# Reordering the first batch of an attention and feed-forward kernel: weight splits and loads tied to slots

## The chip, the cores and the metric

One core of a Trainium2 chip runs the program. The metric is the device time of that core in microseconds (us). Below, PE is TensorE, DVE is VectorE, ACT is ScalarE, POOL is GpSimd, and SP is the SyncE queue that issues every DMA of this kernel.

## The reference

All data are float32. Attention works on q, k, v of shape (4, 8, 576, 64) at two scales and adds the results; two feed-forward layers follow on x of shape (2304, 512).

```python
# coarse: mean over 4 neighbours of q, k and v, full softmax attention on 144 tokens, each row repeated 4 times
out_up = repeat(softmax(scale * q_d @ k_d.T) @ v_d, 4)
# local: softmax over the keys with |i - j| < 4
out_local = softmax(where(mask, scale * q @ k.T, -1e9)) @ v
x = (out_up + out_local)                 # to (2304, 512)
h = x @ w_in1;  y = maximum(0.01 * h, h) @ w_out1
h = y @ w_in2;  out = (h - tanh(h)) @ w_out2      # w_in 512 x 2048, w_out 2048 x 512
```

## The kernel before

**Pairs of heads.** The 32 heads form 16 pairs. One pair's attention is cut into 17 steps, 0 to 16, each a few instructions on each engine (the functions `attention` of the five blocks). Steps 0 to 3 transpose q and k on PE and copy them to SBUF on ACT; step 4 puts the mask and the local scores into two PSUM banks (PE), and DVE takes the maximum of the first; step 5 subtracts the maxima (DVE), and its first subtraction frees bank 0; step 6 is the coarse scores (PE) and the sum of v over 4 neighbours (POOL, three additions, `vd`); step 7 is the maximum of the coarse scores (DVE) and the exponential of the local ones (ACT, L679); step 8 the coarse exponential (ACT, L683) and the local row sums (DVE, L944 to L948); steps 9 and 10 the multiplications by 1/sum (POOL, L1112 and L1117); steps 11 to 14 transpose the probabilities (PE, L451, L456) and copy them (ACT, for some DVE); steps 15 and 16 are the products with v (PE), and DVE adds the two scales into xT.

**The first batch.** Before any feed-forward work can start, the four pairs A, B, C and D4 (written D in the text) of batch 0 run together. Each has a place for its tiles and two PSUM banks. The generator `batch0` (L260) writes out their order on every engine: in slot t pair A is at step t, B at step t-4, C at t-8, D at t-12; within a slot the steps below 6 come first, then falling step numbers. A dictionary, another one for each engine, moves single steps: `(A, 6): (B, 3)` puts A's step 6 behind B's step 3. A name such as C4 below is step 4 of pair C. Every engine works in order, so this order is what an instruction can be stuck behind; semaphores guard the tiles and banks.

**Feed-forward layer 1.** It runs over 8 tiles of 288 tokens. In each tile f runs over 16 slices of 128 hidden units: `hidden1` is w_in times x, `down1` is w_out times the activation, two slices behind. Each product is three float32r products of high and low parts (hi*hi, hi*lo, lo*hi). The high part of a weight is a copy by ACT (`split_kept`, L708), the low part a subtraction by POOL (L1121). Slices 0 to 7 (`KEPT`) are split once and kept, written K0 to K7 for ACT and k0 to k7 for POOL below; 8 to 15 are split again in each tile. K0 and K1 are split within the first batch (`EARLY = 2`), K2 right behind it, K3 to K7 in tile 0. The first tile's x is split too (`split_first_x` on ACT, L733, `lo_of_first_x` on DVE, L976), one part for each pair A to D. During tiles 0 to 5 the attention of two further pairs is threaded between the slices (`later`, L275), all in place A; the first of them is "pair 1" of A.

**Loads.** SP issues all loads in a fixed order (L360 to L387): q and k, v in two layouts (`v4n` for the coarse scale, `vw` for the local one), and the weight slices (`load_kept`, two DMAs of 256 KB each). `load_kept(f)` waits until POOL is done with slice f-4, and `load_whole(0)` until DVE is done with pairs C and D.

**Fillers.** PE begins with 8 throw-away matmuls (`fill`, L630), and five further places of the batch have one or two.

Of the kernel before, what the change touches and what calls it, by code (L numbers as in the profile page):

```python
# [59 lines left out]
def two_scale_attention_and_feed_forward(nc, q, k, v, w_in1, w_out1, w_in2, w_out2, out):  # L60
# [36 lines left out]
    with ExitStack() as ctx:  # L97
# [161 lines left out]

        def batch0(behind):  # L260

            def placed(at, s):
                yield at, s
                for (moved, step), place in behind.items():
                    if place == (s, at):
                        yield from placed(step, moved)

            for slot in range(STEPS + 3 * BEHIND):
                places = [(slot - BEHIND * c, s) for c, s in enumerate(FIRST)
                          if 0 <= slot - BEHIND * c < STEPS]  # L270
                for at, s in sorted(places, key=lambda place: (place[0] % STEPS >= 6, -(place[0] % STEPS))):
                    if (s, at) not in behind:
                        yield from placed(at, s)

        def later(f, tile, last):  # L275

# [34 lines left out]
        def _(sp):  # L311
# [62 lines left out]
            load_qk(A, 1, 8)  # L374
            load_kept(2)
# [40 lines left out]
        def _(pe):  # L416
# [246 lines left out]
        def _(act):  # L663
# [185 lines left out]
            act.wait_ge(band_copied, 1)  # L849
            copy_band(top, 2, NB - 1, 1).then_inc(band_copied, 1)  # L850
            act.wait_ge(zeros_set, 1)
            for step, s in batch0({(A, 8): (C, 1), (A, 11): (B, 7), (A, 12): (B, 8), (A, 15): (C, 8), (B, 11): (C, 7), (B, 12): (C, 8),
                                   (D4, 7): (B, 14), (C, 15): (D4, 11)}):
                attention(step, s, 0)
                if (s, step) == (B, 7):
                    split_kept(0)
                elif (s, step) == (D4, 8):
                    split_kept(1)
                elif (s, step) == (D4, 11):
                    split_first_x(0)  # L860
                elif (s, step) == (D4, 13):
                    split_first_x(1)
                elif (s, step) == (D4, 15):
                    split_first_x(2)
# [26 lines left out]
        def _(dve):  # L891
# [171 lines left out]
            last.then_inc(zeros_set, 1)  # L1063
            dve.wait_ge(zeros_set, 1)
            dve.wait_ge(band_copied, 2)
            for step, s in batch0({(A, 8): (B, 5), (B, 8): (C, 5), (C, 12): (D4, 8), (D4, 9): (C, 12),
                                   (A, 15): (C, 14), (A, 16): (A, 15), (B, 15): (D4, 12), (B, 16): (B, 15),
                                   (C, 15): (B, 16), (C, 16): (D4, 14)}):
                attention(step, s, 0, 0, FIRST.index(s))
                if (s, step) == (D4, 15):  # L1070
                    lo_of_first_x(0)
                    lo_of_first_x(1)
            lo_of_first_x(2)
# [22 lines left out]
        def _(pool):  # L1096
# [129 lines left out]
```

## Time and profile before

| What | Value |
| --- | --- |
| time, median of 3 runs | 953.15 us (952.77 to 954.95) |
| the profiled execution | 954.95 us, its span 953.2 us |
| PE busy | 940.0 us (99% of the span) |
| DVE, ACT, POOL busy | 538.8, 558.4, 403.3 us |
| DMA over the span | 41.48 MB, mean 44 GB/s |
| DMA over the first 60 us | 11.25 MB, mean 188 GB/s |

The span begins with the first recorded instruction. A busy engine is not an engine at its peak, and a share over the whole span says little on the first 70 us, where the change is; the rows are therefore taken from there.

### The profile page before, as it was taken

How to read it: one execution, taken by the hardware profiler on the slowest of the kernel's cores; microseconds unless marked ns; L12 is line 12 of the kernel's file. 1: busy time of each engine (PE TensorE's matmuls, PEld its weight loads, DVE VectorE, ACT ScalarE, POOL GpSimd, SP SyncE). 2: the span in 40 equal slices, each digit the busy share in tenths (PEclk: the TensorE clock that was granted, in tenths of full speed). 3: DMA queues.
4: the chain of work that ended last, by engine and by line, in shares of the span. 5: the costliest groups of instructions: out<-in, count | busy, mean ns of one | idle time of the engine just before them, and what ended most of it. 6: DMA issues, size and time to landing. Idle time of an engine off the chain costs nothing.

```text
span 953.2 us, 19930 instructions
## 1 busy us (share of the span) xinstructions
PE 940.0 (99%) x7026; PEld 883.5 (93%) x7026; DVE 538.8 (57%) x1078; ACT 558.4 (59%) x1351; POOL 403.3 (42%) x343
## 2 busy tenths in 40 slices
PE   8989999999999999999999999999999999999998
PEld 8789999999999999999999989899899898898997
DVE  6745445534544554453236576776666766766764
ACT  5655546445445455464446687666666756756754
POOL 4675517227245155171433667332233233233232
PEclk9999999999999999999999999999999999999999
DMA  7785111210221121102004012000000000000000
GB/s 160 178 209 140 39 39 28 51 32 20 49 51 26 25 51 36 41 3 67 1 2 128 17 57 88 21 14 1 34 0 0 33 0 0 33 0 0 34 1 33
DMA packets 87797, 41.48 MB, mean 44 GB/s; under 512 B 60352, under 2 KB 81344, under 8 KB 87744
## 3 DMA queue, kind: packets, MB, share of 16 engines
q1 hardware_dynamic: 87744, 40.78, 16.4%
q8 instruction: 33, 0.54, 0.2%
q14 instruction: 20, 0.16, 0.1%
HBM read 36.04 MB, written 4.72 MB: 43 GB/s over the span
## 4 chain that ended last, share of the span: by engine, by line
PE 88%; POOL 3%; ACT 3%; DMA 2%; issue 1%; SPq 1%; DVE 1%; ACTq 0%; POOLq 0%; DVEq 0%
PE ph L538 13%; PE ph L539 13%; PE ph L540 13%; PE acc L567 7%; PE acc L568 7%; PE acc L569 7%; PE acc L614 6%; PE acc L615 6%; PE acc L616 6%; PE banks L427 2%; PE banks L464 2%; PE banks L420 1%; POOL g_lo L1149 1%; PE banks L451 1%; POOL w_lo_b L1156 1%
## 5 line engine op out<-in xcount | busy, mean ns | idle before, releaser
L1149 POOL TENSOR_TENSOR g_lo<-scratch,g_hi 128x384 fp32r<-128x384 f32 x96 | 125.6, 1308 | 258.1 <-ACT g_hi L741 258.1
L996 DVE TENSOR_TENSOR ph<-g,ph 128x288 f32<-128x288 f32 x128 | 59.1, 462 | 169.2 <-ACT g L755 168.6
L538 PE MATMUL ph<-x_hi,w_hi_a 128*128 128x288 f32 (+1 forms) x448 | 143.7, 321 | 0.2
L540 PE MATMUL ph<-x_hi,w_lo_a 128*128 128x288 f32 (+1 forms) x448 | 140.0, 312 | 0.0
L539 PE MATMUL ph<-x_lo,w_hi_a 128*128 128x288 f32 (+1 forms) x448 | 139.9, 312 | 0.0
L1128 POOL TENSOR_TENSOR in_lo<-w_whole,in_hi 128x512 fp32r<-128x512 f32 x64 | 82.5, 1289 | 132.3 <-ACT in_hi L721 131.5
L755 ACT ACTIVATE g<-ph 128x288 f32<-128x288 f32 x128 | 52.6, 411 | 134.5 <-PE ph L540 134.5
L1133 POOL TENSOR_TENSOR out_lo<-w_whole,out_hi 128x512 fp32r<-128x512 f32 x64 | 86.2, 1347 | 71.8 <-ACT out_hi L725 71.7
L1030 DVE SCALAR_TENSOR_TENSOR scratch<-scratch,ph 128x384 f32<-128x384 f32 x96 | 53.2, 554 | 108.9 <-ACT scratch L804 104.3
L803 ACT ACTIVATE scratch<-ph 128x384 f32<-128x384 f32 x96 | 46.8, 488 | 108.2 <-PE ph L540 106.7
L983 DVE TENSOR_TENSOR g_lo<-ph,g_hi 128x288 fp32r<-128x288 f32 x128 | 58.6, 458 | 59.3 <-ACT g_hi L741 59.3
L538 PEld LDWEIGHTS ph<-x_hi,w_hi_a 128*128 128x128 f32 x448 | 84.3, 188 | 3.3 <-issue 0.6
L539 PEld LDWEIGHTS ph<-x_lo,w_hi_a 128*128 128x128 f32 x448 | 84.2, 188 | 1.4
L540 PEld LDWEIGHTS ph<-x_hi,w_lo_a 128*128 128x128 f32 x448 | 84.2, 188 | 0.0
L538 PE MATMUL ph<-x_hi,in_hi 128*128 128x288 f32 x256 | 79.1, 309 | 0.0
L567 PE MATMUL acc<-g_hi,out_hi 128*128 128x288 f32 x256 | 76.9, 300 | 0.5 <-POOL out_lo L1133 0.5
L568 PE MATMUL acc<-g_lo,w_hi_a 128*128 128x288 f32 x256 | 75.7, 296 | 0.0
L568 PE MATMUL acc<-g_lo,out_hi 128*128 128x288 f32 x256 | 75.7, 296 | 0.0
L569 PE MATMUL acc<-g_hi,out_lo 128*128 128x288 f32 x256 | 75.7, 296 | 0.0
L567 PE MATMUL acc<-g_hi,w_hi_a 128*128 128x288 f32 x256 | 75.6, 295 | 0.0
L539 PE MATMUL ph<-x_lo,in_hi 128*128 128x288 f32 x256 | 75.5, 295 | 0.0
L569 PE MATMUL acc<-g_hi,w_lo_a 128*128 128x288 f32 x256 | 75.5, 295 | 0.0
(273 smaller groups left out, 2638.1 us busy)
## 6 DMA issues: line engine op xcount, KB each, us to landing
out_dram<-o_stage SPq DMA_DIRECT2D x18, 256.0 KB, 2.0
w_whole<-in_moe_w_in_dram SPq DMA_DIRECT2D x16, 256.0 KB, 4.2
w_whole<-in_moe_w_out_dram SPq DMA_DIRECT2D x16, 256.0 KB, 5.1
qn<-in_q_dram SPq DMA_DIRECT2D x26, 144.0 KB
kn<-in_k_dram SPq DMA_DIRECT2D x26, 144.0 KB
v4n<-in_v_dram SPq DMA_DIRECT2D x26, 144.0 KB
vw<-in_v_dram SPq DMA_DIRECT2D x26, 122.5 KB
scratch<-in_moe_w_in_dram SPq DMA_DIRECT2D x8, 256.0 KB, 2.8
```

Source lines behind the costliest of these rows:

```text
L538: pe.matmul(bank, whi, x_hi[:, c, 0:width], start=(c == 0), stop=False)
L539: pe.matmul(bank, whi, x_lo[:, c, 0:width], start=False, stop=False)
L540: last = pe.matmul(bank, wlo, x_hi[:, c, 0:width], start=False, stop=(c == CD - 1))
L567: pe.matmul(acc[:, c, 0:T1], whi, g1_hi[:, f % 3, :], start=(f == 0), stop=False)
L568: pe.matmul(acc[:, c, 0:T1], whi, g1_lo[:, f % 3, :], start=False, stop=False)
L569: last = pe.matmul(acc[:, c, 0:T1], wlo, g1_hi[:, f % 3, :], start=False, stop=(f == CF - 1))
L614: pe.matmul(acc[:, j, 0:DM], hi, whi, start=(f == 0), stop=False)
L983: dve.tensor_tensor(g1_lo[:, f % 3, :], ph1[:, 1 - f % 2, 0:T1], g1_hi[:, f % 3, :].bitcast(F32), ALU.subtract).then_inc(g_lo_done, 1)
L996: dve.tensor_tensor(ph1[:, 1 - f % 2, 0:T1], g1[:, f % 2, :], ph1[:, 1 - f % 2, 0:T1], ALU.max)\
L1128: pool.tensor_tensor(in_lo[:, f % 2, :], w_whole[:, f - KEPT, 0:DM], in_hi[:, f % 2, :].bitcast(F32), ALU.subtract).then_inc(in_lo_done, 1)
L1133: pool.tensor_tensor(out_lo[:, f % 2, :], w_whole[:, f - KEPT, DM:CW], out_hi[:, f % 2, :].bitcast(F32), ALU.subtract).then_inc(out_lo_don ...
L1149: pool.tensor_tensor(g2_lo[:, f % 3, :], g2[:, f % 2, :], g2_hi[:, f % 3, :].bitcast(F32), ALU.subtract).then_inc(g_lo_done, 1)
```

## The change

The dictionaries of PE, ACT, DVE and POOL lose most of their entries, `batch0` yields the slot number as well, and the splits of K0 and K1, k0 and k1, and of the first x are tied to the beginning of slots. SP issues the first two weight slices later. The fillers are the same, at the same steps.

```diff
+KEPT_HI_SLOTS = (22, 26)
+KEPT_LO_SLOTS = (24, 27)
+FILL = {("a", 1): 2, ("a", 3): 2, ("b", 1): 1, ("b", 3): 2, ("c", 3): 2}
+X_HI_SLOTS = {27: (0, 1), 28: (2,)}
+X_LO_SLOTS = {27: (0, 1), 28: (2,)}
@@ SP
             load_v4(B, 0, 2)
-            load_kept(0)
             load_qk(D4, 0, 6)
-            load_vw(A, 0, 0)
             load_v4(C, 0, 4)
             load_v4(D4, 0, 6)
+            load_vw(A, 0, 0)
             load_vw(B, 0, 2)
+            load_kept(0)
+            load_vw(C, 0, 4)
             load_kept(1)
-            load_vw(C, 0, 4)
             load_vw(D4, 0, 6)
@@ PE
-            for step, s in batch0({(A, 6): (B, 3), (B, 6): (C, 3), (C, 6): (D4, 3), (A, 11): (C, 4), (A, 15): (D4, 4),
-                                   (B, 11): (D4, 4), (C, 15): (D4, 12), (C, 16): (D4, 14)}):
+            for _, step, s, i in batch0({(A, 11): (C, 4), (B, 11): (D4, 4), (C, 15): (D4, 12), (C, 16): (D4, 14)}):
@@ ACT
-            for step, s in batch0({(A, 8): (C, 1), (A, 11): (B, 7), (A, 12): (B, 8), (A, 15): (C, 8), (B, 11): (C, 7), (B, 12): (C, 8),
-                                   (D4, 7): (B, 14), (C, 15): (D4, 11)}):
-                attention(step, s, 0)
-                if (s, step) == (B, 7):
-                    split_kept(0)
-                elif (s, step) == (D4, 8):
-                    split_kept(1)
-                elif (s, step) == (D4, 11):
-                    split_first_x(0)
...
+            for slot, step, s, i in batch0({(D4, 7): (B, 15), (C, 15): (D4, 11)}):
+                if slot != done:
+                    for c in X_HI_SLOTS.get(slot, ()):
+                        split_first_x(c)
+                if slot != done and kept_at(KEPT_HI_SLOTS, slot) is not None:
+                    split_kept(kept_at(KEPT_HI_SLOTS, slot))
+                done = slot
+                attention(step, s, i)
@@ DVE
-            for step, s in batch0({(A, 8): (B, 5), (B, 8): (C, 5), (C, 12): (D4, 8), (D4, 9): (C, 12),
-                                   (A, 15): (C, 14), (A, 16): (A, 15), (B, 15): (D4, 12), (B, 16): (B, 15),
-                                   (C, 15): (B, 16), (C, 16): (D4, 14)}):
...
+            for slot, step, s, i in batch0({(C, 12): (D4, 9), (A, 15): (C, 14), (A, 16): (A, 15),
+                                            (B, 15): (D4, 12), (B, 16): (B, 15), (C, 15): (B, 16),
+                                            (C, 16): (D4, 14)}):
@@ POOL
-            for step, s in batch0({(B, 6): (A, 6), (D4, 6): (C, 9)}):
-                attention(step, s, 0)
-                if (s, step) == (A, 10):
-                    split_kept(0)
-            for f in range(1, EARLY + 1):
-                split_kept(f)
+            for slot, step, s, i in batch0({(D4, 6): (D4, 10)}):
+                if slot != done and kept_at(KEPT_LO_SLOTS, slot) is not None:
+                    split_kept(kept_at(KEPT_LO_SLOTS, slot))
...
+            split_kept(EARLY)
```

Written out from slot 6 on, the orders are these (f: fillers; x0 to x3, l0 to l3: high and low parts of the first x):

```
PE   before: B2 B3 f A6 B4 C0 C1 C2 C3 f B6 C4 A11 D0 A12 D1 A13 D2 A14 D3 C6 D4 A15 B11 A16 B12 B13 B14 D6 B15 C11 B16 ...
PE   after:  B2 A6 B3 f B4 C0 C1 C2 B6 C3 f C4 A11 D0 A12 D1 A13 D2 A14 C6 D3 A15 D4 B11 A16 B12 B13 B14 D6 B15 C11 B16 ...
ACT  before: B3 A7 C0 C1 A8 C2 C3 B7 K0 A11 D0 B8 A12 D1 A13 D2 A14 D3 C7 B11 C8 A15 B12 B13 B14 D7 B15 C11 D8 K1 C13 D11 x0 C15 D13 x1 D15 x2 x3
ACT  after:  B3 A7 C0 A8 C1 C2 C3 A11 B7 D0 A12 B8 D1 A13 D2 A14 D3 A15 B11 C7 B12 C8 B13 B14 B15 D7 C11 D8 C13 K0 D11 C15 D13 K1 x0 x1 D15 x2 x3
DVE  before: A5 B3 A7 B4 B5 A8 A9 C3 B7 C4 C5 B8 B9 D3 C7 D4 C8 D5 C9 D7 D8 C12 D9 C14 A15 A16 D12 B15 B16 C15 D14 C16 D15 l0 l1 D16 l2 l3
DVE  after:  A5 B3 A7 B4 A8 B5 A9 C3 B7 C4 B8 C5 B9 D3 C7 D4 C8 D5 C9 D7 D8 D9 C12 C14 A15 A16 D12 B15 B16 C15 D14 C16 l0 l1 D15 l2 D16 l3
POOL before: A6 B6 A9 A10 k0 B9 B10 C6 C9 D6 C10 D9 D10 k1 k2
POOL after:  A6 A9 A10 B6 B9 B10 C6 C9 C10 D9 D10 D6 k0 k1 k2
```

## Rows read from the trace of the kernel before

**Rows 1.** Windows: us, then busy us (instructions), PE clock, DMA share, GB/s.
```profile
43.00:60.00 17.00, 16.32 (x149) 15.37 (x148) 9.94 (x21) 10.52 (x24) 10.47 (x7) 1.00 1.01 247
60.00:72.00 12.00, 9.77 (x83) 8.97 (x83) 3.95 (x9) 6.37 (x14) 8.69 (x6) 1.00 0.61 148
72.00:90.00 18.00, 18.00 (x195) 17.67 (x192) 8.85 (x19) 8.81 (x20) 10.50 (x10) 1.00 0.70 185
```
**Rows 2.** Waits of PE in 0 to 150 us: total, times, longest.
```profile
PE banks L451 <- POOL pl L1112: 2.4, 2, 1.8
...
PE banks L446 <- ACT kT L673: 0.7, 1, 0.7
...
PE banks L451 <- ACT pT L688: 0.4, 1, 0.4
```
**Rows 3.** Timeline of PE: start, length, line, operation [idle before].
```profile
5.12 1.21 PE L420 MATMUL banks<-ident,qn 72*128 72x72 f32 x8
...
13.86 0.90 PE L503 MATMUL banks<-kdT,qd_diag 128*96 128x144 f32 x6
...
16.27 0.72 PE L420 MATMUL acc<-ident,turned_c 72*128 72x72 f32 x8
...
19.66 1.38 PE L427 MATMUL acc<-kT_c,qT_c 64*64 64x70 f32 x36
21.55 0.63 PE L451 MATMUL banks<-ident,pl 128*70 128x128 f32 x4 [0.52 <-POOL pl L1112]
...
26.82 1.38 PE L427 MATMUL ph<-kT_d,qT_d 64*64 64x70 f32 x36
...
37.00 0.44 PE L456 MATMUL acc<-ident,pd_c 96*72 96x96 f32 x3 [0.42 <-DVE turned_c L957]
...
42.49 0.72 PE L420 MATMUL banks<-ident,qn 72*128 72x72 f32 x8
```
**Rows 4.** Timeline of DVE, columns as in Rows 3.
```profile
13.11 0.51 DVE L929 TENSOR_TENSOR pl<-banks,mxl 128x350 f32<-128x350 f32 x1
...
17.64 0.51 DVE L929 TENSOR_TENSOR xT<-acc,xT 128x350 f32<-128x350 f32 x1
...
18.92 0.80 DVE L944 TENSOR_REDUCE rs<-pl 128x9 f32<-128x630 f32 x1
...
29.53 0.80 DVE L944 TENSOR_REDUCE rs_c<-pl_c 128x9 f32<-128x630 f32 x1
```
**Rows 5.** Timeline of ACT.
```profile
19.10 0.73 ACT L679 ACTIVATE xT<-xT 128x630 f32<-128x630 f32 x1
...
26.23 0.76 ACT L679 ACTIVATE pl_c<-pl_c 128x630 f32<-128x630 f32 x1
...
45.34 1.06 ACT L710 ACTIVATE w_hi_a<-w_whole 128x1024 fp32r<-128x1024 f32 x1 [0.71 <-DMA w_whole<-in_moe_w_out_dram]
...
53.27 1.06 ACT L710 ACTIVATE w_hi_a<-w_whole 128x1024 fp32r<-128x1024 f32 x1 [2.31 <-DMA w_whole<-in_moe_w_out_dram]
...
64.27 1.06 ACT L710 ACTIVATE w_hi_a<-w_whole 128x1024 fp32r<-128x1024 f32 x1 [4.29 <-DMA w_whole<-in_moe_w_out_dram]
```
**Rows 6.** Timeline of POOL.
```profile
22.32 2.36 POOL L1123 TENSOR_TENSOR w_lo_a<-w_whole,w_hi_a 128x1024 fp32r<-128x1024 f32 x1
...
32.97 1.53 POOL L1105 TENSOR_TENSOR vd_d<-vd_d,v4n_d 72x256 f32<-72x256 f32 x2
...
61.16 1.24 POOL L1112 TENSOR_TENSOR pl<-pl,rs 128x630 f32<-128x630 f32 x1
```
**Rows 7.** Timeline of the SP queue: issue start, length.
```profile
13.48 0.41 SPq L344 DMA_DIRECT2D w_whole<-in_moe_w_in_dram  x1
...
16.18 2.63 SPq L317 DMA_DIRECT2D turned_d<-in_k_dram  x2
...
36.00 1.72 SPq L315 DMA_DIRECT2D qn<-in_q_dram  x2
...
56.66 0.87 SPq L346 DMA_DIRECT2D w_whole<-in_moe_w_out_dram  x1
```

More of the change, by code:

```diff
@@ L85, in two_scale_attention_and_feed_forward @@
     WHOLE = CF - KEPT
+    EARLY = len(KEPT_HI_SLOTS)
     assert D == QB and DM == CD * P and LP * RUN == S and NB * QB == S and PAIRS == 4 + 2 * MIXED
@@ L260, in batch0, with placed @@
         def batch0(behind):
-            def placed(at, s):
-                yield at, s
+            def placed(slot, at, s):
+                yield slot, at, s, 0
                 for (moved, step), place in behind.items():
                     if place == (s, at):
-                        yield from placed(step, moved)
+                        yield from placed(slot, step, moved)
             for slot in range(STEPS + 3 * BEHIND):
@@ L272, in batch0, with kept_at @@
                     if (s, at) not in behind:
-                        yield from placed(at, s)
+                        yield from placed(slot, at, s)
+        def kept_at(slots, slot):
+            return slots.index(slot) if slot in slots else None
         def later(f, tile, last):
@@ L636, in _ @@
             fill(8, ph1[:, 1, :])
-            fills = {(A, 1): 2, (A, 3): 2, (B, 1): 1, (B, 3): 2, (C, 3): 2}
-            for step, s in batch0({(A, 6): (B, 3), (B, 6): (C, 3), (C, 6): (D4, 3), (A, 11): (C, 4), (A, 15): (D4, 4),
-                                   (B, 11): (D4, 4), (C, 15): (D4, 12), (C, 16): (D4, 14)}):
-                attention(step, s, 0)
-                fill(fills.get((s, step), 0), ph1[:, 1, :])
+            for _, step, s, i in batch0({(A, 11): (C, 4), (B, 11): (D4, 4), (C, 15): (D4, 12), (C, 16): (D4, 14)}):
+                attention(step, s, i)
+                fill(FILL.get(("abcd"[FIRST.index(s)], step), 0), ph1[:, 1, :])
             for step in range(HEAD):
@@ L851, in _ @@
             act.wait_ge(zeros_set, 1)
-            for step, s in batch0({(A, 8): (C, 1), (A, 11): (B, 7), (A, 12): (B, 8), (A, 15): (C, 8), (B, 11): (C, 7), (B, 12): (C, 8),
-                                   (D4, 7): (B, 14), (C, 15): (D4, 11)}):
-                attention(step, s, 0)
-                if (s, step) == (B, 7):
-                    split_kept(0)
-                elif (s, step) == (D4, 8):
-                    split_kept(1)
-                elif (s, step) == (D4, 11):
-                    split_first_x(0)
[L861 to L864, printed above, removed]
+            done = -1
+            for slot, step, s, i in batch0({(D4, 7): (B, 15), (C, 15): (D4, 11)}):
[5 more added lines that the diff above has]
+                done = slot
+                attention(step, s, i)
             split_first_x(CD - 1)
@@ L1065, in _ @@
             dve.wait_ge(band_copied, 2)
-            for step, s in batch0({(A, 8): (B, 5), (B, 8): (C, 5), (C, 12): (D4, 8), (D4, 9): (C, 12),
-                                   (A, 15): (C, 14), (A, 16): (A, 15), (B, 15): (D4, 12), (B, 16): (B, 15),
-                                   (C, 15): (B, 16), (C, 16): (D4, 14)}):
[L1069 to L1073, printed above, removed]
+            done = -1
+            for slot, step, s, i in batch0({(C, 12): (D4, 9), (A, 15): (C, 14), (A, 16): (A, 15),
+                                            (B, 15): (D4, 12), (B, 16): (B, 15), (C, 15): (B, 16),
+                                            (C, 16): (D4, 14)}):
+                if slot != done:
+                    for c in X_LO_SLOTS.get(slot, ()):
+                        lo_of_first_x(c)
+                done = slot
+                attention(step, s, i, i, FIRST.index(s))
             lo_of_first_x(CD - 1)
@@ L1183, in _ @@
                 pool.memset(s.vw[:, 0:NB:NB - 1, :, :], 0.0).then_inc(vw_zeroed, 1)
-            for step, s in batch0({(B, 6): (A, 6), (D4, 6): (C, 9)}):
-                attention(step, s, 0)
-                if (s, step) == (A, 10):
-                    split_kept(0)
-            for f in range(1, EARLY + 1):
-                split_kept(f)
+            done = -1
+            for slot, step, s, i in batch0({(D4, 6): (D4, 10)}):
+                if slot != done and kept_at(KEPT_LO_SLOTS, slot) is not None:
+                    split_kept(kept_at(KEPT_LO_SLOTS, slot))
+                done = slot
+                attention(step, s, i)
+            split_kept(EARLY)
             layer1(0, CF)
```

1 line of the change is left out of this document (removed).

## The prediction

> **What bounds the kernel now.** I began with the table by windows, since a share over 953 us can't speak for an edit to the first 43. From 72 us on PE is busy without a hole (18.00 of 18.00), at a granted clock of 1.00, the 2.4 GHz level [rows 1]. Whatever comes out of the change must therefore move the moment at which PE enters this dense run. Then the waits of PE, to see what stands before it. Behind the first batch there are three: 0.7 for a copy of k, 1.8 for a multiplication by POOL, 0.4 for a copy of the probabilities, 2.9 us together [rows 2]; the windows agree (0.7 idle in 43 to 60, 2.2 in 60 to 72). Last the timelines, for what these waits hang on: ACT is in order, and its splits K2, K4 and K6 start when their DMA has landed, at 45.34, 53.27 and 64.27, after 0.71, 2.31 and 4.29 us of idleness [rows 5]. The DMA engines are full from 43 to 60 (share 1.01, 247 GB/s) [rows 1]. So the kernel has two racing paths to about 67 us: the first batch on the engines, and the weights through SP and DMA. The second one ends last; the first has some slack. That is the hinge of this prediction.
>
> **The change in the first batch.** I follow the new order with the lengths of the rows; ends and starts are some 0.05 to 0.15 us apart, as between 13.11 + 0.51 = 13.62 [rows 4] and the start at 13.86 behind the fillers.
>
> Step 1, A6 ahead of B3 on PE. A6 waits for the first subtraction of A5, which ends at 13.62 [rows 4]; it used to wait behind B3 and two fillers instead. It starts near 13.7, takes 0.65, then come B3 (0.25) and the fillers (0.5), so B4 starts at 15.1, and C0, which stood at 16.27 [rows 3], at 16.9: 0.6 late. DVE's B4 is late by 0.5 with it.
>
> Step 2, A8 ahead of B5 on DVE, and B6 ahead of C3 on PE. A8 (sum, epsilon, reciprocal, 1.26 us) runs from 18.1 instead of 18.92 [rows 4], so POOL can multiply 0.8 earlier. But B5's first subtraction goes from 17.64 [rows 4] to 19.3, it ends at 19.8, and it frees the bank that B6 waits for. PE has done C2 at 18.0 and stands at B6 until 19.9, with C3, the fillers and C4 queued behind. C3 ends at 20.8, the fillers at 21.3, and C4's masks and scores (1.8) at 23.1, against 19.66 + 1.31 = 20.97 before [rows 3]: 2.1 late. A11 follows at 23.1 instead of 21.55 [rows 3].
>
> Step 3, ACT. The exponential B7, at 19.10 before [rows 5], now stands behind A11 and runs from 24.1 to 24.8. DVE's B8 waits for it until 24.9 and C5, now behind B8, runs from 26.1; C6 on PE then from 26.7. ACT's D3 comes at 28.0, D4's scores on PE from 29.3 to 30.6, against 26.82 to 28.12 [rows 3]. The exponential C7, 26.23 before [rows 5], now stands behind B11, which needs PE after D4: it ends at 32.4, and DVE's C8 starts at 32.5 against 29.53 [rows 4], 2.9 late. D5, D7, D8 follow; DVE's copy C12, now behind D9, starts at 38.8, and PE's C14, which waits for it, at 39.5 against 37.00 [rows 3]. From there the order on PE is the old one, so that pair 1's A0, 42.49 before [rows 3], comes at about 45.0. The delay at the end of the batch is 2.5 us.
>
> Bounds of this step: the order removes nothing from any engine. PE's waits inside the batch are the ceiling of a gain: 0.52 and 0.42 in the rows and some 2.7 in all by its timeline, so -2.7. Above, the stalls of steps 1 to 3 with no overlap add up to 0.6 + 1.9 + 0.6 + 0.7 + 1.1 = 4.9. I take 2.5, the walk.
>
> Step 4, the tail. POOL's D6 (0.7 + 1.53 [rows 6]) moves behind D10; PE's D15 waits for it. D10 ends at 40.4 in the walk, D6 at 42.7, and D15 is due at 43.3: hidden by 0.6. k0 (2.36 [rows 6]) then ends at 45.1 and k1 at 47.5; the first slice on PE is due at 45.5 and ends when the last low part of x is ready, near 47.1, the second is due at 48.1: hidden by 0.4 and 0.6. K0, K1 and the x parts fill holes of ACT, except K1 ahead of x0, which is hidden because x3 waits for D16 anyway.
>
> Step 5, the loads. SP issues without a pause, so the same issues in another order reach A's next q at 36.00 [rows 7] again. K0, issued at 13.48 [rows 7], goes to about 27.5 and K1 to 31.8; ACT needs them at 39 and 42.6 now. D's q and k land earlier, but PE's D0 stands behind A11 and gains nothing. Vw of A is issued some 0.7 later and needed at 28, by A15. Cost zero; bounds -1 to +1, since a pair of like issues took 2.63 us at 16.18 and 1.72 at 36.00 [rows 7]: the queue can back up by 0.9 in one place, and the order decides where. The waits of later loads hold too: the fifth kept slice needs k0 by 47, which is done at 45.1.
>
> **What the DMA path absorbs.** ACT's K2 waits 0.71 for its DMA [rows 5], so a delay of 2.5 is 1.8 to 1.9 from there on, and PE's wait of 0.7 [rows 2] is its mirror. At K4 ACT has 2.31 of idleness [rows 5]: all 1.9 is swallowed on ACT. On DVE it is not: pair 1's A4 and A5 end 1.9 later, at 55.7, and the activation maximum that stood at 54.66 now waits for them, 1.0 late. That runs on through the coarse maximum, ACT, k5 and POOL's multiplication at 61.16 [rows 6], so that PE's A11 starts 1.0 after its old 62.5. PE itself arrives there at 62.4, so it waits 1.1 instead of 1.8. Then A13: before, it waited 0.4 for a copy that stood behind K6 on ACT, itself held by the landing at 64.25 of the DMA issued at 56.66 [rows 2, 5, 7]. This landing doesn't move. PE comes 1.0 late and 0.4 is absorbed: 0.6 us enters the dense run, and there is no slack in it to take it away or add to it.
>
> The sum: 2.5 - 0.7 - 0.8 - 0.4 = +0.6 us. On the profiled execution's own 954.95 (span 953.2 and 1.75 around it) that is 955.55; that execution was 1.8 above the median of the runs, so I set it on the median, 953.15 + 0.6 = 953.8. More generally the result is the delay of the batch less about 2, and never below zero unless the DMA comes earlier.
>
> **A rule of the skill.** Across the wait of 1.8 at 60.6 [rows 2] the granted clock stays 1.00 [rows 1], though the eight transposes at 5.12 took 1.21 us and the like ones at 16.27 took 0.72 [rows 3], so PE did begin slower than it goes on. The Trainium skill, "TensorE: Matmul & The Clock Gate", Part 1 (The HAM clock gate), says that activity releases the throttle and that idleness brings it back, half the pace. By that rule the new stall in front of B6 could do harm well beyond its length; by the row of the wait at 60.6, of the same length, it does none. The sum goes by the row.
>
> **The rivals.**
> (a) PE falls back to the slow pace behind the new stalls (18.0 to 19.9, and again near 26 and 38). For: the slow first transposes; the new stalls stand closer together than any before. Against: the wait of 1.8 did no harm. Place: C3 to B11, some 10 us of PE; at 1.21 against 0.72 [rows 3] the work of about 6 us grows by 4, the batch is 6.5 late, and the total +4.5: 957.6. It decides from a batch delay of 4 on, below that the waits for DMA take it up.
> (b) The reorder pays: POOL, DVE and the earlier loads of v and D overlap better than I see, and the batch is not late. For: A8 is 0.8 earlier. Against: B6's bank. Time: nothing is gained, since A13 still waits for K6: 953.15, within 0.2%.
> (c) DMA comes earlier: the kept slices out of the congested early queue make SP quicker, K4 and K6 land up to 2 us earlier, and the batch isn't late. The most that can go are the 2.9 us of waits [rows 2]: 950.3. Against: the engines are full from 43 to 60, and SP's issues are the same.
> (d) The queue backs up more, or the new tail on POOL (D6, k0, k1 in a row) shows: each further microsecond there goes straight to the first slices. With 2 more the batch is 4.5 late: +2.6, 955.7.
>
> **How the numbers follow.** A difference of 0.2%, 1.9 us, is about what a measurement of this kernel tells from none. The forecast (a delay of 1.5 to 3.8 at the batch's end, 0 to +1.8 in total) gets 0.53, (b) 0.15, (a) 0.07, (d) 0.14, (c) 0.11. (d) and (a) are slower by over 0.2% but for 0.02 of (d): 0.19. (c) is faster by over 0.2%: 0.11, less 0.01 of it that falls short: 0.10. Same: 0.71. The range reaches from 951.3, within (c), to 956.8, past (d); the likeliest case alone is 953.15 to 955.0.
>
> **What would show it.** In the changed kernel's timeline PE waits some 1.9 us before B6 near 18 to 20; DVE's B8 and C8 wait for ACT's exponential; A0 of pair 1 starts near 45. K4 and K6 still start at 53.3 and 64.3 after DMA; PE's wait for POOL's multiplication shrinks from 1.8 to about 1.1, the two others to nothing, and from 72 us on PE is dense. The prediction is wrong if K6 starts more than 1 us off 64.3, if A0 comes before 43 or after 46.5, or if a wait of PE appears behind 72 us.

## The result and the profile after

The changed kernel takes 959.66 us (median, 958.63 to 960.50), the kernel before beside it on the same chips 953.55 (952.77 to 954.95): a ratio of 1.0062 with a 95% interval of [1.0044, 1.0080]. The prediction said 953.8 with a range up to 956.8. The profiled execution took 958.32, its span is 956.5.

The windows (length, then busy us (instructions) of PE, PEld, DVE, ACT and POOL, PE clock, DMA share, GB/s), two of the first batch and the three of [rows 1]:

```profile
12.00:20.00 8.00, 6.04 (x74) 5.40 (x75) 6.96 (x16) 3.35 (x12) 3.84 (x5) 0.93 0.93 171
20.00:28.00 8.00, 7.06 (x82) 6.21 (x80) 5.45 (x14) 4.52 (x16) 3.87 (x5) 0.85 0.89 153
...
43.00:60.00 17.00, 15.07 (x190) 14.21 (x190) 12.83 (x25) 9.92 (x23) 12.26 (x9) 0.90 1.00 284
60.00:72.00 12.00, 11.81 (x93) 11.56 (x92) 5.97 (x13) 8.28 (x20) 10.84 (x6) 1.00 0.47 117
72.00:90.00 18.00, 18.00 (x199) 17.50 (x198) 6.66 (x14) 8.73 (x21) 8.37 (x8) 1.00 0.56 160
```

From 72 us on nothing has changed in kind: 18.00 of 18.00 busy, clock 1.00. What changed lies before. In 12 to 28 and in 43 to 60 the mean granted clock is below 1, so a part of each stretch was spent at 1.2 GHz.

The waits of PE (total, times, longest), against [rows 2]:

```profile
PE ph L546 <- DVE xT L897: 1.9, 1, 1.9
PE acc L464 <- DVE turned_c L959: 1.9, 1, 1.9
PE acc L511 <- DVE xT L931: 1.6, 1, 1.6
```

The three long waits of before, for kT, pl and pT, are gone or are 0.2 us. In their place stand B6 (L511), C14 (L464) and the first slice of layer 1 (L546). They are in the timeline of PE, which answers to [rows 3]:

```profile
5.12 0.75 PE L428 MATMUL banks<-ident,qn 72*128 72x72 f32 x8
...
15.37 0.72 PE L428 MATMUL acc<-ident,turned_c 72*128 72x72 f32 x8
...
18.49 1.32 PE L511 MATMUL acc<-xT 128*96 128x144 f32 x6 [1.62 <-DVE xT L931]
...
21.69 1.66 PE L435 MATMUL acc<-kT_c,qT_c 64*64 64x70 f32 x36
23.29 0.63 PE L459 MATMUL banks<-ident,pl 128*70 128x128 f32 x4
...
29.61 1.38 PE L435 MATMUL ph<-kT_d,qT_d 64*64 64x70 f32 x36
...
40.89 0.44 PE L464 MATMUL acc<-ident,pd_c 96*72 96x96 f32 x3 [1.88 <-DVE turned_c L959]
...
46.39 0.72 PE L428 MATMUL banks<-ident,qn 72*128 72x72 f32 x8
49.04 0.40 PE L546 MATMUL ph<-x_hi,w_hi_a 128*128 128x288 f32 x1 [1.93 <-DVE xT L897]
...
67.01 1.07 PE L459 MATMUL banks<-ident,pl 128*70 128x128 f32 x8 [0.19 <-POOL pl L1115]
71.10 0.27 PE L459 MATMUL banks<-ident,pl 128*70 128x128 f32 x1
```

C0 starts at 15.37, 0.9 earlier than in the trace of before. That is not the order's doing: kernels that are the same up to there have it at 15.37 (the change) and 17.31 (fill_three below), since PE's first transposes and fillers ran slowly for a shorter or a longer time (0.75 for the first transposes in the change, 1.21 or 1.22 in before and fill_three). Stretches are therefore counted from C0. From there to pair 1's A0, at 46.39, PE needs 31.02 us instead of 26.22. The last row, step A13 at 71.10, opens the dense run: in this and every other trace of the study the span ends 885.2 to 886.7 us behind A13. So one moment carries the whole result, and the experiments are read by it.

DVE and ACT show what the waits hang on:

```profile
39.00 1.05 DVE L954 TENSOR_SCALAR rs_d<-rs_d 96x3 f32<-96x3 f32 x1 [0.29 <-ACT pd_d L689]
...
40.18 0.66 DVE L959 COPY turned_c<-acc 70x512 f32<-70x512 f32 x1
...
45.50 3.35 DVE L980 TENSOR_TENSOR x_lo<-xT,x_hi 128x288 fp32r<-128x288 f32 x2
```
```profile
24.45 0.72 ACT L685 ACTIVATE xT<-xT 128x630 f32<-128x630 f32 x1
...
32.08 0.72 ACT L685 ACTIVATE pl_c<-pl_c 128x630 f32<-128x630 f32 x1
...
56.20 1.05 ACT L716 ACTIVATE w_hi_a<-w_whole 128x1024 fp32r<-128x1024 f32 x1
...
64.40 1.05 ACT L716 ACTIVATE w_hi_a<-w_whole 128x1024 fp32r<-128x1024 f32 x1
```
```profile
38.79 1.24 POOL L1115 TENSOR_TENSOR pl_d<-pl_d,rs_d 128x630 f32<-128x630 f32 x1 [2.16 <-DVE rs_d L950]
...
43.49 4.67 POOL L1126 TENSOR_TENSOR w_lo_a<-w_whole,w_hi_a 128x1024 fp32r<-128x1024 f32 x2
```

On DVE a tiny operation on 96 x 3 takes 1.05 us and ends with POOL's multiplication (40.05 and 40.03); its like in other places takes 0.20. The first two low parts of x take 3.35 while POOL computes k0 and k1, and the second of them ends at 48.85, 0.69 behind POOL's k1 (43.49 + 4.67 = 48.16). On ACT the exponentials B7 and C7 are 5.4 and 5.9 later than in [rows 5], and K4 and K6 (56.20, 64.40) no longer wait for their DMA.

### The profile page after: what moved, and what is told of

Read it like the earlier page. It is cut to its first block, busy times and chain, and to the rows that moved or that the text cites. A ratio compares the mean times of both kernels' runs of the same rounds, so it can differ in the third digit from the quotient of the medians.

```text
span 956.5 us, 19930 instructions
## 1 busy us (share of the span) xinstructions
PE 940.8 (98%) x7026; PEld 884.6 (92%) x7026; DVE 541.5 (57%) x1078; ACT 558.0 (58%) x1351; POOL 403.2 (42%) x343
## 4 chain that ended last, share of the span: by engine, by line
PE 89%; POOL 3%; ACT 3%; DMA 2%; issue 1%; DVE 1%; SPq 0%; ACTq 0%; DVEq 0%; POOLq 0%
PE ph L546 14%; PE ph L547 13%; PE ph L548 13%; PE acc L575 7%; PE acc L576 7%; PE acc L577 7%; PE acc L622 6%; PE acc L623 6%; PE acc L624 6%; PE banks L435 2%; PE banks L472 2%; PE banks L459 1%; PE banks L428 1%; POOL g_lo L1152 1%; POOL w_lo_b L1159 1%
## 5 line engine op out<-in xcount | busy, mean ns | idle before, releaser
L546 PE MATMUL ph<-x_hi,w_hi_a 128*128 128x288 f32 (+1 forms) x448 | 144.1, 322 | 2.1 <-DVE xT L897 1.9
L546 PEld LDWEIGHTS ph<-x_hi,w_hi_a 128*128 128x128 f32 x448 | 84.7, 189 | 5.2 <-DVE xT L897 2.1
L546 PE MATMUL ph<-x_hi,in_hi 128*128 128x288 f32 x256 | 79.1, 309 | 0.0
L747 ACT ACTIVATE g_hi<-ph 128x288 fp32r<-128x288 f32 x128 | 52.8, 412 | 39.2 <-DVE ph L998 36.6
```

What stands on the lines that cost most here:

```text
L546: pe.matmul(bank, whi, x_hi[:, c, 0:width], start=(c == 0), stop=False)
```

## The experiments

Executions of one kernel differ in their mean granted clock, and an execution at 0.996 or less is as a rule longer than one at 0.998 or more; between 0.998 and 1.0 the clock doesn't order the times. Where this matters the clock is given. "Orders" are the written orders of PE, ACT and DVE; "tail" is the rest: D6, k0, k1 behind D10 on POOL, the places of K0, K1 and of x, and the loads. Each ratio is against the kernel before on the same chip. The median of before differs from chip to chip (952.50 to 953.85), so times of different rows are compared by their ratios.

| run | what it is | median us (n) | ratio [95%] |
|---|---|---|---|
| core_only | before, new orders | 963.11 (6) | 1.0096 [1.0073, 1.0120] |
| tail_only | after, old orders | 954.56 (11) | 1.0013 [1.0004, 1.0021] |
| short_lo | after, k0 and k1 cut | 960.87 (6) | 1.0074 [1.0053, 1.0096] |
| fill_c2 | after, 6 fillers behind C2 | 959.85 (6) | 1.0065 [1.0050, 1.0081] |
| pe_only | before, PE's new order | 954.66 (12) | 0.9993 [0.9974, 1.0013] |
| dve_only | before, DVE's new order | 953.52 (12) | 1.0003 [0.9995, 1.0012] |
| pe_dve | before, both | 955.19 (11) | 1.0017 [1.0008, 1.0025] |
| fill_three | after, 21 fillers in three places | 957.63 (5) | 1.0040 [1.0027, 1.0053] |
| act_only | before, ACT's new order | 954.56 (11) | 1.0020 [1.0012, 1.0029] |
| act_old | after, ACT's old order | 956.28 (5) | 1.0039 [1.0026, 1.0052] |
| fill_short | fill_three, k0 and k1 cut | 956.68 (6) | 1.0044 [1.0029, 1.0060] |
| loads_early | before, other order of later loads | 952.52 (12) | 1.0006 [0.9986, 1.0026] |
| core_fill | core_only, 13 fillers in two places | 957.03 (5) | 1.0042 [1.0029, 1.0055] |
| fix_b6 | after, B6 and A8 back | 959.90 (6) | 1.0069 [1.0049, 1.0088] |
| fix_c12 | after, C12 ahead of D9 | 959.72 (6) | 1.0071 [1.0057, 1.0085] |
| tail_short | tail_only, k0 and k1 cut | 953.43 (11) | 1.0001 [0.9992, 1.0011] |
| loads_fill | loads_early, 3 fillers behind C4 | 952.34 (12) | 0.9981 [0.9962, 1.0000] |

### Orders or tail

My theory behind the result was: the orders stall PE, the stalls cost clock, and k0 and k1 hold up DVE. Rivals were the tail on POOL and the loads.

**core_only**: before.py with the three new tables of places.

```
-  ACT: batch0({(A, 8): (C, 1), (A, 11): (B, 7), ... (D4, 7): (B, 14), (C, 15): (D4, 11)})
+  ACT: batch0({(D4, 7): (B, 15), (C, 15): (D4, 11)})      and PE's and DVE's as in the change
```

> The kernel before with only the new dictionaries of PE, ACT and DVE; POOL's order, SP's loads and the places of K0, K1, the x parts stay as before. Theory 'orders' (the stalls in the batch, B6 above all, with the slow pace of PE behind them, are the loss): most of the 6.1 us, 957 to 960. Theory 'tail' (k0 and k1 late on POOL hold the low parts of x on DVE): the delay of the batch is taken up by the waits for DMA, 953 to 954.5.

**tail_only**: the change with the three old tables.

```
+  PE, ACT, DVE: the tables of before; all else as changed
```

> The changed kernel with the old dictionaries of PE, ACT and DVE: left of the change are POOL's order (D6, k0, k1 late), the slots of K0, K1, x0 to x3, l0 to l3, and SP's loads. Theory 'tail': 3 us or more slower than before, 956.5 to 959, and the two low parts of x on DVE take 3 us or more instead of 0.8. Theory 'orders': within 1 us of before, 952.5 to 954.5.

Core_only loses more than the whole change by the medians (963.11), though the two intervals overlap; tail_only loses 1.3 us, a little more than its theory 'orders' allowed. The orders are the main cause. What no expectation had is the spread of core_only: its six executions took 957.43, 958.27, 963.07, 963.16, 965.22 and 965.92 at mean clocks of 0.998, 0.996, 0.989, 0.989, 0.986 and 0.986. The only window up to 72 us in which the clock goes, in the fastest of them:

```profile
20.00:28.00 8.00, 6.67 (x75) 5.82 (x74) 5.85 (x13) 3.85 (x9) 2.39 (x3) 0.79 0.89 174
```

**short_lo**: POOL computes 64 of the 1024 columns of k0 and k1 (the other columns of these low parts are left out and are zero, which takes one memset more on POOL at the start).

```
+                cut = slice(0, 64 if f < EARLY else CW)
+                pool.tensor_tensor(w_lo_a(f, cut), w_whole[:, WHOLE - 4 + f % 4, cut], ...
```

> The changed kernel with k0 and k1 cut to 64 of 1024 columns on POOL (the rest of the two low parts is left at zero, so that part of the computation is left out). Theory 'tail': the two low parts of x take 0.8 us again instead of 3.35, the first slice of layer 1 starts 2.5 to 3 us earlier and the time is 2 to 3 us under that of the changed kernel, about 957. Theory 'orders': DVE's x parts as before, but the time moves by less than 1 us, 958.7 to 960.5.

**fill_c2**: six fillers behind C2, where PE stands before B6.

```
-FILL = {("a", 1): 2, ("a", 3): 2, ("b", 1): 1, ("b", 3): 2, ("c", 3): 2}
+FILL = {("a", 1): 2, ("a", 3): 2, ("b", 1): 1, ("b", 3): 2, ("c", 2): 6, ("c", 3): 2}
```

> The changed kernel with 6 fillers on PE behind C2, where PE otherwise waits 1.6 us for B6. Theory 'clock' (the stall there lets the clock fall, granted 0.93 and 0.85 in 12 to 28 us): the clock is 1.00 in 12 to 28 us, the batch ends 1.5 to 2.5 us earlier, and since the dense run of PE starts with it, 957.5 to 958.5. If the stalls alone cost, nothing or up to +0.3 us on 959.7.

Neither helps: short_lo lies above both branches of its expectation, fill_c2 where the stalls alone would have it. In short_lo the time again follows the clock (956.78 and 957.84 at 0.998, 960.84 and 960.90 at 0.991, 962.34 at 0.989, 964.30 at 0.986), so its median says nothing of k0 and k1. Its trace does: the low parts take 0.82, the wait before the first slice is gone, the clock is 1.00 from 43 us on, and A13 comes 21.82 behind A0 instead of 24.71. In fill_c2 the clock is 1.00 where the fillers are, and falls later:

```profile
12.00:20.00 8.00, 7.11 (x90) 6.16 (x87) 6.99 (x14) 4.39 (x14) 2.36 (x4) 1.00 0.90 184
20.00:28.00 8.00, 6.83 (x85) 5.97 (x85) 6.78 (x16) 4.11 (x14) 5.13 (x6) 1.00 0.85 143
...
36.00:43.00 7.00, 5.12 (x66) 4.25 (x67) 4.71 (x11) 4.27 (x14) 4.31 (x5) 0.89 0.76 202
43.00:52.00 9.00, 7.55 (x115) 6.20 (x113) 6.82 (x13) 4.04 (x12) 5.54 (x4) 0.90 0.77 200
```

### Which engine's order

**pe_only**, **dve_only** and **pe_dve** put one or two of the tables into the kernel before.

```
-  PE:  batch0({(A, 6): (B, 3), (B, 6): (C, 3), (C, 6): (D4, 3), (A, 11): (C, 4), (A, 15): (D4, 4), ...})
+  PE:  batch0({(A, 11): (C, 4), (B, 11): (D4, 4), (C, 15): (D4, 12), (C, 16): (D4, 14)})
```

> The kernel before with PE's new dictionary alone. DVE still does B5 ahead of A8, so B6 waits little behind C2. Theory 'order and clock' (a long stall of PE needs both orders, and the clock falls only behind a long stall): C0 and all behind it 0.6 us late, clock at least 0.998, 953 to 954.5. Theory 'PE's order alone': over 956.

```
-  DVE: batch0({(A, 8): (B, 5), (B, 8): (C, 5), (C, 12): (D4, 8), (D4, 9): (C, 12), (A, 15): (C, 14), ...})
+  DVE: batch0({(C, 12): (D4, 9), (A, 15): (C, 14), ...})
```

> The kernel before with DVE's new dictionary alone: B5 stands behind A8, and PE does C3 and the fillers before it waits for B6, so that stall is about 0.9 us. Theory 'order and clock': 953 to 955, clock at least 0.996. Theory 'DVE's order alone': over 956.

```
+  both
```

> The kernel before with the new dictionaries of PE and DVE; ACT as before, so the exponentials B7 and C7 come early. If the stall before B6 and the clock behind it are the loss: 956 to 960 with a mean clock under 0.996. If ACT's order is needed as well: 953.5 to 955.5.

**act_only** is the kernel before with ACT's new table alone, **act_old** the change with ACT's old one.

```
-  ACT: batch0({(A, 8): (C, 1), (A, 11): (B, 7), (A, 12): (B, 8), (A, 15): (C, 8), (B, 11): (C, 7), ...})
+  ACT: batch0({(D4, 7): (B, 15), (C, 15): (D4, 11)})
```

> The kernel before with ACT's new dictionary alone, so that A11's copy stands ahead of the exponential B7 and B11's ahead of C7. Theory 'ACT' (the in-order coupling of the exponentials to PE's transposes is what turns the batch late): 956 us or more and a mean clock of 0.996 or less. Theory 'coupling' (ACT's order costs only where PE's and DVE's orders have already made C4 late): 953 to 955.

```
+  the reverse, in the changed kernel
```

> The changed kernel with ACT's old dictionary. Both theories: faster than the changed kernel. By the sum of what was measured (1.7 for PE's and DVE's orders, 1.3 for the tail) 956.0 to 957.0; if ACT's order has no part, 959.7.

DVE's order alone costs nothing, PE's alone next to nothing (its interval is wide because one execution of before took 964.18, at a clock of 0.984; the medians are 1.2 apart), ACT's alone +2.1, PE's and DVE's +1.7; all three cost 9.9. They don't add up: by the medians the parts alone come to 3.3. Act_old agrees with ACT's share: at 1.0039 it is 2.3 us better than the change, give or take 1.4. (Its 956.28 lies in the expected range, but on a chip where before takes 952.50; by the ratio it is just above it.) The exponentials B7 and C7 show how the delays hang together, in pe_dve:

```profile
20.58 0.71 ACT L678 ACTIVATE xT<-xT 128x630 f32<-128x630 f32 x1
27.41 0.70 ACT L678 ACTIVATE pl_c<-pl_c 128x630 f32<-128x630 f32 x1
```

and in the changed kernel at 24.45 and 32.08. With PE's and DVE's orders, in which A8 goes ahead of B5, B7 is 1.5 later than in [rows 5]. With ACT's order too, B7 is queued behind A11, which needs PE after C4: another 3.9. In act_only, ACT's order alone puts B7 at 22.88, 3.8 later than in [rows 5]. So the delays of B7 add up (1.5 and 3.8 against 5.4), and the step from 3.3 to 9.9 us must come from elsewhere; "The clock, taken out" below finds it.

In dve_only A0 comes at 43.67 and A13 at 65.65:

```profile
43.67 0.72 PE L420 MATMUL banks<-ident,qn 72*128 72x72 f32 x8
...
65.65 0.27 PE L451 MATMUL banks<-ident,pl 128*70 128x128 f32 x1
```
```profile
62.07 1.06 ACT L710 ACTIVATE w_hi_a<-w_whole 128x1024 fp32r<-128x1024 f32 x1 [3.01 <-DMA w_whole<-in_moe_w_out_dram]
```

A0 is 1.2 later than in [rows 3] and A13 1.4 earlier, since K6, which starts when its DMA has landed, does so at 62.07 and not at 64.27. Seven traces have K6 waiting for this landing: pe_only and act_only at 62.45, tail_only 62.66 and tail_short 62.84 stand with dve_only's, pe_dve at 64.57 with that of before, although SP's order is the same in before, dve_only, pe_only, act_only and pe_dve. So the row of before that I used is one of the two late ones. Part of the lateness is there when SP issues the load: at 56.66 in before and 58.55 in pe_dve, against 55.70, 56.79 and 55.44 in dve_only, pe_only and act_only; from the issue to K6's start it is 7.6 and 6.0 against 6.4, 5.7 and 7.0. What holds the queue back, and how much of it is chance, one trace of each kernel can't tell.

### The clock, taken out

**fill_three**: fillers in all three places in which PE waits.

```
+FILL: ("c", 2): 6
+                if (s, step) == (C, 13):
+                    pe.wait_ge(D4.bank_free[1], uses1(0, 3))
+                    fill(7, ph1[:, 1, :])
+            pe.wait_ge(B.bank_free[0], uses0(1, 0))      # ahead of the first slice
+            fill(8, acc[:, 0, :])
```

> The changed kernel with fillers in all three of its long stalls of PE: 6 behind C2, 7 behind C13, 8 ahead of the first slice of layer 1. Theory 'clock': the granted clock is 1.00 in every window up to 72 us, the mean 0.998 or more in every execution, and the time falls to 954.5 to 957, what is left being the stalls themselves. Theory 'stalls': 959 to 960.5 as in the changed kernel.

**fill_short**: the same with k0 and k1 cut as in short_lo.

```
+                cut = slice(0, 64 if f < EARLY else CW)      # in fill_three
```

> The changed kernel with fillers in its three long stalls and with k0 and k1 cut to 64 of 1024 columns (the rest of these low parts is left at zero). With the clock held at its full level the effect of POOL's splits on DVE's x parts can be read: theory 'tail' says the two parts take 0.8 us instead of 3.4 and the time falls from 957.6 by 1 to 2 us, to 955.6 to 956.6. If POOL's splits don't hold DVE: 957.6.

**core_fill**: core_only with the fillers behind C2 and C13.

```
+ fills[(C, 2)] = 6, and behind C13: pe.wait_ge(D4.bank_free[1], uses1(0, 3)); fill(7, ph1[:, 1, :])
```

> The three new dictionaries alone (as core_only, 963.1) with 6 fillers behind C2 and 7 behind C13. Theory 'clock': mean clock 0.998 or more in nearly every execution and 955.5 to 957.5, so that 5 us or more of that kernel's loss is the pace. If the orders themselves cost it: 960 or more.

With fillers core_only goes from 963.11 to 957.03, its clock is 1.0 in four executions of five, and 13 useless matmuls have made the kernel 6 us faster by the medians (5 us by the ratios, give or take 3, since core_only spreads so widely). The window and A0 and A13:

```profile
20.00:28.00 8.00, 6.39 (x83) 5.37 (x82) 7.49 (x16) 5.59 (x17) 4.56 (x4) 1.00 0.90 167
```
```profile
46.41 0.72 PE L420 MATMUL banks<-ident,qn 72*128 72x72 f32 x8
...
68.24 0.27 PE L451 MATMUL banks<-ident,pl 128*70 128x128 f32 x1
```

The change itself goes from 1.0062 to 1.0040 in fill_three, 2.1 us; the difference has an uncertainty of 1.8 us, so in the change the clock's price is likely and its size open. The medians leave fill_three 0.6 above what was expected. What is left at full clock, +3.6 in core_fill and +3.8 to +4.1 in fill_three (by medians 957.63 to 953.50), is the delay proper. The 3.6 is near the 3.3 of the three tables alone: what did not add up there was the clock.

Fill_short has 1.0044, on another chip: cutting k0 and k1 shows nothing in the time there, and its expectation missed. Its trace says why it could hardly show more. The low parts are ready at 46.82, but the eight fillers now hold PE until 49.20:

```profile
47.45 2.00 PE L641 MATMUL acc<-ident 128*128 128x128 f32 x16
49.20 0.38 PE L546 MATMUL ph<-x_hi,w_hi_a 128*128 128x288 f32 x1
```

### One stall at a time

**fix_b6** puts B6 back behind C3 and A8 behind B5; **fix_c12** puts C12 back ahead of D9.

```
-  PE:  batch0({(A, 11): (C, 4), ...            DVE: batch0({(C, 12): (D4, 9), ...
+  PE:  batch0({(B, 6): (C, 3), (A, 11): (C, 4), ...    DVE: batch0({(A, 8): (B, 5), (C, 12): (D4, 9), ...
```

> The changed kernel with B6 behind C3 on PE and A8 behind B5 on DVE, as before the change, everything else changed. The stall of 1.6 us before B6 goes. Theory 'B6' (that stall and the slow pace behind it are the largest part): 956 to 957.5. Theory 'ACT chain' (the exponentials behind A11 and B11 set the pace whatever B6 does): 958.5 or more.

```
-  DVE: batch0({(C, 12): (D4, 9), ...
+  DVE: batch0({(C, 12): (D4, 8), (D4, 9): (C, 12), ...
```

> The changed kernel with DVE's copy C12 ahead of D9, as before the change. The stall of 1.9 us before C14 goes. Theory 'each stall counts' 957.5 to 958.7; if the path through the exponential D8 sets the end anyway, 959.3 to 960.

Neither is better than the change, at 1.0069 and 1.0071: the theories 'B6' and 'each stall counts' are out, and the times fall where the other branch of each expectation had them. In fix_b6 the stall before B6 is gone from the trace, and the clock is worse than ever in it:

```profile
28.00:36.00 8.00, 8.00 (x85) 6.50 (x86) 3.67 (x8) 2.42 (x7) 2.11 (x3) 0.50 0.76 199
...
43.00:52.00 9.00, 9.00 (x108) 7.88 (x106) 6.28 (x14) 3.69 (x9) 6.73 (x5) 0.54 0.76 186
52.00:60.00 8.00, 8.00 (x76) 7.79 (x75) 3.57 (x7) 5.17 (x12) 3.55 (x2) 0.67 0.93 292
```

PE is busy for all 8.00 us of 28 to 36, at half the speed (this execution took 962.42, the second longest of its six). In fix_c12 the wait before C14 falls from 1.88 to 0.42 and that before the first slice grows from 1.93 to 2.96: the stall moved.

```profile
39.35 0.44 PE L464 MATMUL acc<-ident,pd_c 96*72 96x96 f32 x3 [0.42 <-DVE turned_c L959]
...
48.97 0.41 PE L546 MATMUL ph<-x_hi,w_hi_a 128*128 128x288 f32 x1 [2.96 <-DVE xT L897]
```

DVE's low parts and POOL's k0 and k1 in the same trace:

```profile
44.36 4.42 DVE L980 TENSOR_TENSOR x_lo<-xT,x_hi 128x288 fp32r<-128x288 f32 x2
```
```profile
43.42 4.67 POOL L1126 TENSOR_TENSOR w_lo_a<-w_whole,w_hi_a 128x1024 fp32r<-128x1024 f32 x2
```

DVE began its low parts 1.1 earlier than in the change and ended them at the same moment, 48.78 against 48.85, and A13 stayed (71.04 against 71.10). The end hangs on POOL: in all seven traces with whole k0 and k1 at their new place (after, tail_only, act_old, fill_c2, fill_three, fix_b6, fix_c12) the second low part ends 0.68 or 0.69 behind k1, although A0 stands anywhere from 40.93 to 51.53. So in the change's trace the path that ends last goes through POOL: D10, D6, k0, k1, then the low parts, the first slice, A13. The end of the batch, A0, stands beside it.

### k0, k1 and DVE

**tail_short**: tail_only with k0 and k1 cut as in short_lo.

```
+                cut = slice(0, 64 if f < EARLY else CW)      # in tail_only
```

> The changed tail and loads with the old dictionaries (as tail_only, 954.6), k0 and k1 cut to 64 of 1024 columns on POOL, the rest of these low parts at zero. Theory 'shared path of DVE and POOL': the two low parts of x take 0.8 us instead of 4.2, PE's wait of 2.8 before the first slice goes, mean clock 0.998 to 1.0, 952.8 to 953.8, nothing left of the 1.3 us. If not: 954.6.

Here the clock is 0.998 to 1.0 and the spread is small: 1.0013 [1.0004, 1.0021] becomes 1.0001 [0.9992, 1.0011], on two chips, a difference of 1.1 us with an uncertainty of 1.0. DVE's first two low parts in tail_only and, with nearly nothing to do for POOL, in tail_short:

```profile
40.05 4.23 DVE L982 TENSOR_TENSOR x_lo<-xT,x_hi 128x288 fp32r<-128x288 f32 x2
```
```profile
40.11 0.81 DVE L982 TENSOR_TENSOR x_lo<-xT,x_hi 128x288 fp32r<-128x288 f32 x2
```

In tail_only PE waits 2.82 us before the first slice, and the clock is 0.81 in 43 to 52; in tail_short's trace the clock is 1.0. The 1.1 us are therefore DVE's hold with the clock that it costs, together.

### The loads, and a faster kernel

**loads_early**: the kernel before, with A's next v and vw between the kept slices.

```
-            load_v(A, 1, 8)
-            for j in range(WHOLE - 4): load_whole(j)
+            load_v4(A, 1, 8)        # behind K5; vw behind K7, then the whole slices
```

> The kernel before with another order of SP's loads behind the third kept slice: slices 4 and 5, v4n of pair 1, slices 6 and 7, vw of pair 1, then the four whole ones. Theory 'two paths' (the DMA of K4 and K6 sets when the dense run begins): K4 and K6 no longer wait for DMA, the 1.8 and 0.4 us waits of PE shrink, and the time is 1.5 to 2.5 us less, 951 to 952. If the dense run is set by the batch: 953.5.

**loads_fill**: that with three fillers behind C4.

```
-            fills = {(A, 1): 2, (A, 3): 2, (B, 1): 1, (B, 3): 2, (C, 3): 2}
+            fills = {(A, 1): 2, (A, 3): 2, (B, 1): 1, (B, 3): 2, (C, 3): 2, (C, 4): 3}
```

> The kernel before with the early weight loads (as loads_early) and three more fillers behind C4, where PE waits for POOL ahead of A11. Theory 'two floors' (the dense run begins at the later of the batch's end plus 21.8 us and the landing of K6 plus 2.8): pair 1's A0 near 41.5, the part of A13 that waits near 63.3, 949.5 to 951.5, faster than both kernels. If the batch's end alone counts: as loads_early with its A0, 951.5 to 953.

Loads_early takes K4's and K6's wait for DMA away (A13 at 65.34); in its trace the batch is slower, with a clock of 0.86 in 20 to 28 and an A0 at 43.50, and the time is the same as before's, where 951 to 952 was expected. With the fillers the clock is 1.0 and A13 comes at 64.85:

```profile
42.86 0.72 PE L421 MATMUL banks<-ident,qn 72*128 72x72 f32 x8
...
64.85 0.27 PE L452 MATMUL banks<-ident,pl 128*70 128x128 f32 x1
```

Its ratio of 0.9981 is the lowest of the study (952.34 against 953.85), but the interval ends at 1.0000: a gain that is likely and not proved. The 949.5 to 951.5 of the theory 'two floors' was missed, and so was its A0, 42.86 instead of about 41.5.

## Why the prediction was wrong

**Where the miss lies.** The forecast of 953.8 puts A13 at 66.0 (less 886 of tail and 1.8 around the span); the trace has it at 71.10. The 5.1 us between are: 0.8 of slack that was no slack (its own A0 of 45.0 with 21.8 behind it is 66.8); 2.9 from C0 to A0, where the walk of steps 1 to 3 had 28.1 and the trace 31.0; less 1.5, because C0 happened to start at 15.37 and not at 16.9; and 2.9 behind A0, where step 4 had nothing. The lost clock, also taken at nothing, is spread over both terms of 2.9.

**The hinge was half right.** PE is dense from A13 on in every trace, and the tail behind it is constant within 1.4 us. So was the list of places: PE stands 1.62 before B6 (1.9 predicted), B7 and C7 are late on ACT, and pl's wait is nearly gone. But in the change neither of the two racing paths ends last: K6 no longer waits for its DMA, and behind A0 PE waits for a path through POOL that was not among the two.

**Step 4, "hidden by 0.4 and 0.6", failed.** It counted when k0 and k1 end, and not what they do to DVE meanwhile: 3.35 us instead of 0.81 for the first two low parts of x, so that the first slice waits 1.93. The walk's own time for POOL was good: k1 was to end at 47.5 and ended at 48.16. With the 0.69 that the low parts end behind it, the 0.19 from there to the first slice and the 21.70 from the first slice to A13 in fill_three, at full clock, 47.5 gives A13 at 70.1 and a time of 957.9; this estimate is made afterwards from rows of other traces. By itself the new tail costs 1.1 to 1.3 us (tail_only, and tail_only against tail_short). The Trainium skill, "GPSIMD Engine Reference", section 1 (Specifications), lists POOL's SBUF interfaces as shared with VectorE, with contention for DVE instructions that have two SBUF inputs. The trace agrees: x_lo reads two tensors in SBUF, and takes 4.23 beside POOL's subtractions and 0.81 without them. On top of the new orders the times don't settle its share: fill_three and fill_short differ by nothing, give or take 1.9, and the fillers of fill_short stand in the way.

**"A rule of the skill" failed as well.** I let one row decide, a wait of 1.8 us after which the clock stayed 1.00 [rows 1, 2], and gave rival (a) 0.07. With waits of like length in the new places the clock is 0.93, 0.85 and 0.90. The Trainium skill, "TensorE: Matmul & The Clock Gate", Part 1 (The HAM clock gate), has it that idleness brings the throttle back; the runs agree, with 963.11 against 957.03 for one and the same order without and with fillers. The row showed that a wait of 1.8 us can be harmless at that place, among work that keeps PE busy. It was no evidence for a stretch with further waits close by. In core_only the clock costs 5 to 6 us; in the change about 2, which is not clear of noise. Rival (a) came nearest in size (957.6) and not in structure: the lost clock doesn't stay with its stall.

**Steps 1 to 3, the walk, were sized too small.** It gave 1.9 from C0 to A0 on top of 26.22; at full clock fill_three needs 29.67 and core_fill 31.13 (46.41 less C0 at 15.28), fillers included, and the change 31.02 with its lost clock. That the walk met B7 well (24.1, measured 24.45) was luck: counted from C0 it had 7.2, and the trace 9.1. It also took DVE's operations at their length when alone: 1.05 instead of 0.20 for D9's, which is 0.85 of the 1.4 by which C14, due at 39.5, was late at 40.89. Step 1's 0.6 was about right: against before's C0 of 16.27, the four traces of changed kernels with a like slow start have 17.12 to 17.31, and of those with a quicker one the new orders have 15.31 to 15.54 (after, act_old, fix_c12) and the old ones 14.47 and 14.80 (tail_only, tail_short). (One length was read as 1.31 where [rows 3] has 1.38; nothing hangs on it.)

**Step 5, the loads at zero, held** within 1 us: tail_short has the changed loads and stands at 1.0001.

**"What the DMA path absorbs" had the right mechanism and an unlucky row.** In the traces of before and of the kernels with its tail, A13 is the later of two floors, A0 + 21.8 (21.83 in core_fill, 21.98 in dve_only) and K6's landing + 2.8 (64.27 and 67.09 before). With whole k0 and k1 in the new tail it comes later than both, by 1.0 in tail_only and 3.9 in fix_c12, which is the path through POOL (in tail_short, without them, by 0.5). In before's profiled execution the second floor stood 2.8 above the first, whose A0 was at 42.49. In five other traces the landing is 62.1 to 62.8, and the slack then ends at an A0 of about 43.5. The late landing is probably also why this execution was 1.8 above the median; that is worked out from the constant tail, and no second trace of before shows it. I took both: the slack of the slow execution, and then its 1.8 off the sum. With a landing of 62.5, my own A0 of 45.0 gives 66.8, and with the constants behind it (886 and 1.8) 954.6 instead of 953.8.

**The sum, seen from the times.** Changed less before is 6.1 us by the medians: 3.6 to 4.1 is delay at full clock, the rest, about 2, is what fillers bring back. Of the profiled execution's A0 to A13 of 24.71, 21.83 is the floor, and 2.9 goes with k0 and k1: short_lo's trace, without them, has 21.82. The clock from the first slice on is 0.4 of it (22.06 against 21.70 in fill_three).

**Still open**: what decides in which stretch the clock falls. Taking one stall away moved it (fill_c2, fix_b6) and did not shorten the kernel. And no run keeps the change's clock up and its first slice free of both POOL and fillers, so how far the times would follow the traces there is not shown.

## What to carry to other kernels

In a start-up phase of in-order engines, an order table is one object: moving a step ahead of its producer on one engine cost 0 to 2 us, on three engines together 10, of which about 4 were delay and the rest lost clock. Where TensorE waits for a microsecond or two in several places near each other, compare the mean granted clock of every execution before explaining any time, and try fillers in all of these places, not in one. But fillers also hold the engine: where another change takes the wait away, take its fillers out, or they hide the gain. Ask of work moved to the end of one engine's list which other engine it slows, and not only when it ends. A slack read from one profiled execution is that execution's; if it ends at a DMA landing, allow for that landing to be 2 us earlier in others, and don't take the same excess off a second time.

## What the hardware showed that I had not expected

Operations of DVE with next to no data can take as long as POOL's neighbour runs: 96 x 3 elements in 1.05 us instead of 0.20, ending 0.02 us behind POOL's multiplication. In thirteen of the traces this operation (D9's first on the coarse sums) takes 0.64 to 1.21 us and ends within 0.03 us of it; in act_old, where it starts as POOL ends, it takes 0.17. And a program's own spread can be its clock: core_only ran from 957.43 to 965.92 with nothing else changed, 8.5 us for a mean clock of 0.998 against 0.986, and the kernel before had single executions at 964.18 with 0.984.
